# Three small TensorE operations cut from full 128-wide shapes to the rows and columns that they use

## The chip, the cores and the metric

The kernel runs on one core of a Trainium2 chip. The metric is the device time of one execution in microseconds (us); lower is better. Engines are named PE (TensorE, with PEld for its weight loads), DVE (VectorE), ACT (ScalarE), POOL (GpSimd) and SP (the queue that issues DMAs).

## The reference

Three parts follow one another. Only the first is touched by the change; here it is, cut to what matters:

```python
# q, k, v: (2, 8, 768, 64) fp32, proj: (64, 6)
q_bucket = bits of (q @ proj > 0);  k_bucket = bits of (k @ proj > 0)
mask = q_bucket[..., :, None] == k_bucket[..., None, :]
scores = where(mask, q @ k.T / 8, -1e9)
scores = scores - max(scores, axis=-1)
attn = exp(scores) / (sum(exp(scores)) + 1e-9)
out = attn @ v                      # 16 heads of 768 x 64
```

Then come `h = max(x@w1, x@w2, x@w3) @ w_out` on 1536 tokens of 512, and an ELU feed-forward network of width 2048.

## The kernel before

All matmuls keep fp32 accuracy by splitting a value into a high part (`fp32r`) and the low remainder, and running three products. In the program this gives triples such as L623, L624, L625.

The attention part handles 16 heads, one per "slot". A slot has 12 steps (6 tiles of 128 keys times 2 halves of 384 queries), and work on several heads is interleaved: in slot s the scores of head s are made (`scores`, L608 and L609, two matmuls a step), the row maxima of head s+1 (`maxima`, L596, 12 a slot), and the weighted values of half 1 of head s-1 and half 0 of head s (`weigh`, L623 to L625, one triple a step). PE executes its queue in the order in which `emit` (L635) writes it; every cross-engine dependence is a semaphore. Slots 4 to 11 are a hardware loop of two passes over four slots, the others are written out.

Three small operations are in question:

- **The turn of the maxima** (L654, once a slot, after step 8). DVE's L485 leaves the maximum of each query row in 12 columns of `row_max`, a tile of 128 columns; the other 116 are zeros from a memset at the start. PE transposes the whole 128x128 tile; DVE's L499 then reads the 12 rows that matter.
- **The sum of the values** (L659, once a slot, right behind it). A matrix of ones, 128x128, times `val_sum` (128x64) puts the sum of all values on 128 partitions; DVE's `value_total` (L541, L543) reads 12 of them.
- **The correction of an empty row** (L632, twice a slot, the last matmul of each half of `weigh`). It adds `total` times `empty` to the accumulated output. Both operands have 128 partitions, of which 14 hold values (12 rows of `ROWS`, one for each of two parts of epsilon); `total` is zero on the others, and these add nothing. Its end (`pv_ready`) lets ACT copy the half out (L357, L358), and PE may begin the next half's accumulation (L623) when that is done.

In the program each matmul also carries the tile of the PE array that it is issued for. It is 128 rows by 64 columns for L625, whose stationary operand has 64 columns, and the full 128 by 128 for every other matmul of the kernel before, L596 with its 96 rows included.

`set_totals` (L425) is DVE's one-time fill of `total`, `empty`, `minus` and `row_max`, in the slot of offset -1; POOL fills `ones` at L323.

Of the kernel before, what the change touches and what calls it, by code (L numbers as in the profile page):

```python
# [28 lines left out]
FP32 = mybir.dt.float32  # L29
FP32R = mybir.dt.float32r  # L30
# [4 lines left out]
B, H, S, D = 2, 8, 768, 64  # L35
# [4 lines left out]
P = 128  # L40
T = S // P
# [81 lines left out]
def attention(nc, q, k, v, proj, w1, w2, w3, xh, xl, raw, wh, wl, banks, w_loaded, w_split, w_ready, f_ready):  # L123
    ctx = ExitStack()
    with ctx:  # L125
# [4 lines left out]
            return ctx.enter_context(nc.semaphore(name))  # L130

        ident = sb("ident", [P, P])
        ones = sb("ones", [P, P])
        neg_block = sb("neg_block", [ROWS, T, P])


# [13 lines left out]

        total = sb("total", [P, 2, 2 * D], FP32R)
        empty = sb("empty", [P, 2, S], FP32R)
        rounded = sb("rounded", [ROWS, D], FP32R)
        minus = sb("minus", [ROWS, 1])

# [14 lines left out]
        p_hi = sb("p_hi", [P, KEPT, HALF], FP32R)  # L172
        p_lo = sb("p_lo", [P, KEPT, HALF], FP32R)
        half_max = sb("half_max", [P, 2, T, 2])
        row_max = sb("row_max", [P, 2, P])
        x = sb("x", [P, 4, HALF])
        inv = sb("inv", [P, 4, HALF])

# [3 lines left out]
        misc = banks[:, RING + 3:, :]  # L182

        turned = {("q", True): misc, ("k", True): banks[:, 0:2, :], ("q", False): misc, ("k", False): misc}
        mt_all = mx_ps[0][:, HALF:HALF + P]
        mt_ps = mt_all[0:ROWS, :]
        sum_all = mx_ps[1][:, HALF:HALF + D]
        sum_ps = sum_all[0:ROWS, :]

        consts = sem("consts")  # L190
        rows_set = sem("rows_set")
# [222 lines left out]
        def _(dve):  # L414
# [10 lines left out]
            def set_totals():  # L425
                dve.memset(empty[:].bitcast(FP32), 1.0).then_inc(rows_set, 1)
                dve.memset(minus[:], -1.0).then_inc(rows_set, 1)
                dve.memset(row_max[:], 0.0).then_inc(rows_set, 1)
                dve.memset(total[:].bitcast(FP32), 0.0).then_inc(rows_set, 1)
                dve.wait_ge(rows_set, 19)  # L430
                dve.memset(minus[0:T, :], 0.0).then_inc(rows_set, 1)
                dve.memset(total[0:ROWS + 2, :, D:2 * D].bitcast(FP32), EPS_LO).then_inc(rows_set, 1)
                dve.wait_ge(rows_set, 21)
                dve.memset(total[0:ROWS + 1, :, D:2 * D].bitcast(FP32), EPS_HI).then_inc(rows_set, 1)
                dve.wait_ge(rows_set, 22)
                dve.memset(total[0:ROWS, :, D:2 * D].bitcast(FP32), 0.0).then_inc(rows_set, 1)
                dve.wait_ge(rows_set, 23)
                dve.memset(total[0:T, :, D:2 * D].bitcast(FP32), float(S)).then_inc(rows_set, 1)

            def low(s, x, n):  # L440
# [19 lines left out]
            def emit(s):  # L460
                m = s.off + 1
                if s.off == FIRST_SLOT + 2:
                    set_totals()
                for n in range(STEPS):
                    if n == MAX_BEFORE[V_AT + 2] and s.has_st:
                        par = s.off % 2
                        dve.wait_ge(vh_done, s.count(1, 1))
                        dve.tensor_tensor(v_lo[:, par, :, :], v_raw[:, par, :, :],
                                          v_hi[:, par, :, 0:D].bitcast(FP32), ALU.subtract).then_inc(vl_done, 1)
                    if n == INV_AT and s.has_unit:  # L470
                        reciprocals(s, 1)

                    if n == (10 if s.off == FIRST_SLOT + 2 else MAX_BEFORE[TP_AT[0] + 3]) and s.has_tp:
                        low(s, "q", 1)
                    if n == MAX_BEFORE[HASH_AT[0] + 1] and s.has_hash:
                        take_bits(s, "q", 1)
                    if n == MAX_BEFORE[HASH_AT[1] + 1] and s.has_hash:
                        take_bits(s, "k", 2)
                    if s.has_max:
                        dve.wait_ge(mx_ready, s.count(STEPS, STEPS + n + 1))  # L480
                        dve.tensor_reduce(half_max[:, m % 2, n // 2, n % 2:n % 2 + 1], mx_ps[n % 2][:, 0:HALF],  # L481
                                          AX.X, ALU.max).then_inc(mx_read, 1)
                if s.has_max:
                    dve.wait_ge(mx_read, s.count(STEPS, 2 * STEPS))
                    dve.tensor_reduce(row_max[:, m % 2, 0:ROWS].rearrange("p (a t) -> p a t", a=2),  # L485
                                      half_max[:, m % 2, :, :].unsqueeze(1).to_broadcast([P, 2, T, 2]), AX.X, ALU.max
                                      ).then_inc(max_done, 1)
                if s.has_unit:
                    reciprocals(s, 0)
                if s.has_st:  # L490
                    value_total(s)
                if s.has_max:

                    dve.wait_ge(mt_ready, s.count(1, 2))
                    if s.off == FIRST_SLOT + 2:
                        dve.wait_ge(consts, 14)
                        dve.wait_ge(rows_set, 24)
                    rows = operands[m % GROUP][96:96 + ROWS, Q1, :]
                    dve.scalar_tensor_tensor(  # L499
                        out=rows.rearrange("p (t n) -> p t n", t=T), in0=mt_ps.unsqueeze(1).to_broadcast([ROWS, T, P]),  # L500
                        scalar=NONE_BELOW, in1=neg_block[:], op0=ALU.max, op1=ALU.mult).then_inc(mrow_done, 1)
                if s.off == FIRST_SLOT:
                    dve.wait_ge(proj_split, 1)
                    dve.tensor_tensor(proj_lo[:], proj_raw[:], proj_hi[:].bitcast(FP32), ALU.subtract
                                      ).then_inc(proj_split, 1)
                if s.has_tp:
                    low(s, "k", 2)
                if s.has_max:
                    value_sum(s)

                    dve.wait_ge(mrow_done, s.count(1, 2))
                    wait(dve, pv_ready, s.count(2))
                    dve.tensor_scalar(empty[0:ROWS, m % 2, :], rows.bitcast(FP32), -0.5 * NONE_BELOW, None, ALU.is_ge
                                      ).then_inc(empty_done, 1)
                if s.off in (HEADS - 1, HEADS + 1):


                    j = max(s.off - HEADS, 0)
                    dve.wait_ge(w_split, j + 1)
                    dve.wait_ge(st_ready, (HEADS - GROUP + 1) * STEPS)  # L520
                    dve.tensor_tensor(wl[:, j, :], raw[:, j, :], wh[:, j, :].bitcast(FP32), ALU.subtract
                                      ).then_inc(w_ready, 1)
# [27 lines left out]
        def _(pe):  # L550
# [84 lines left out]
            def emit(s):  # L635
                for step in range(STEPS):
                    if s.has_st and step % LAG != 1:
                        scores(s, step)
                    if s.has_max:
                        for n in range(MAX_BEFORE[step], MAX_BEFORE[step + 1]):  # L640
                            maxima(s, n)
                    for i, x in enumerate("qk"):
                        if s.has_tp and step == TP_AT[i]:
                            transposes(s, x, i + 1)
                        if s.has_hash and step == HASH_AT[i]:
                            project(s, x, i + 1)
                    if s.has_st and step % LAG == 0:

                        scores(s, step + 1)
                    if s.has_half1 if step < LAG else s.has_half0:  # L650
                        weigh(s, step)
                    if step == TURN_AT and s.has_max:
                        pe.wait_ge(max_done, s.count(1, 2))
                        pe.transpose(mt_all, row_max[:, (s.off + 1) % 2, :], ident[:]).then_inc(mt_ready, 1)  # L654
                    if step == TURN_AT and s.has_st:
                        pe.wait_ge(vsum_done, s.count(1, 1))
                        if s.off == 0:
                            pe.wait_ge(consts, 15)
                        pe.matmul(sum_all, ones[:], val_sum[:], start=True, stop=True).then_inc(sum_ready, 1)  # L659
                if s.off == HEADS:  # L660


                    pe.wait_ge(w_ready, 1)
                    pe.wait_ge(xl_done, HEADS // B)
                    pe.wait_ge(exp_done, HEADS * STEPS)
                    for u, x in EARLY:
                        if (u, x) == (1, 0):
                            pe.wait_ge(w_ready, 2)
                            pe.wait_ge(mrow_done, HEADS)
                            pe.wait_ge(total_done, 2 * HEADS)  # L670
                        expert(pe, banks, wh, wl, xh, xl, u, x, f_ready)
# [424 lines left out]
```

## Time and profile before

| | |
|---|---|
| median of 3 executions | 757.33 us |
| lowest, highest | 757.12, 758.61 us |
| the profiled execution | 758.61 us |
| its span, first to last instruction | 756.8 us |
| mean granted clock of TensorE, share of full speed | 0.98 |

The profile is one execution, the slowest of the three. Its time is 1.8 us more than its span; this lies around the first and last instruction. Attention runs up to about 294 us of the span, the two feed-forward parts behind it. A MATMUL's end in the trace is modelled, so two matmuls in a row overlap in the listing: what a matmul takes of PE is read from the distance of the starts.

### The profile page before, as it was taken

The numbers are of one execution on the slowest core, as the hardware profiler recorded it, in microseconds if no ns is written. First come the engines' busy times: TensorE is split into PE (matmuls) and PEld (weight loads), VectorE is DVE, ScalarE is ACT, GpSimd is POOL, SyncE is SP. The second block draws the span as 40 slices with busy tenths as digits, with TensorE's granted clock in tenths as the row PEclk, the third lists the DMA queues.
The fourth block names the chain that finished last, engine by engine and source line by source line (L and its number), as shares of the span: only waits on it lengthen the run. The fifth ranks groups of instructions, "written<-read, shape, count | busy, mean of one in ns | idle before, by whom it ended". The sixth has DMA issues, their size and how long they took to land.

```text
span 756.8 us, 10421 instructions
## 1 busy us (share of the span) xinstructions
PE 723.3 (96%) x3440; PEld 617.5 (82%) x3440; DVE 386.3 (51%) x611; ACT 406.7 (54%) x802; POOL 387.0 (51%) x348
## 2 busy tenths in 40 slices
PE   4699999989999988999999999999999999999998
PEld 3499988979998877788888888878888888888886
DVE  3677999879898865322222221143434333343433
ACT  1178889868898894122221112165555555565553
POOL 5078889878898997011101001054444444444452
PEclk9599999999999999999999999999999999999999
DMA  6756364563616300211000001032334333343331
GB/s 133 167 136 151 86 134 99 119 152 77 134 29 144 94 1 0 84 42 42 22 0 22 22 21 42 29 108 86 105 92 145 107 100 95 98 153 97 99 98 55
DMA packets 79634, 64.74 MB, mean 86 GB/s; under 512 B 29152, under 2 KB 68832, under 8 KB 79584
## 3 DMA queue, kind: packets, MB, share of 16 engines
q1 hardware_dynamic: 79584, 64.12, 33.1%
q8 instruction: 25, 0.41, 0.2%
q14 instruction: 25, 0.20, 0.1%
HBM read 40.91 MB, written 3.15 MB: 58 GB/s over the span
## 4 chain that ended last, share of the span: by engine, by line
PE 58%; DVE 0%; ACT 0%; issue 0%
PE banks L694 14%; PE banks L696 14%; PE banks L695 14%; PE banks L1037 6%; PE banks L1041 6%; PE banks L1038 6%; DVE g_sb L980 0%; DVE g_sb L976 0%; DVE out_sb L950 0%; ACT gh L935 0%; ACT neg L930 0%
## 5 line engine op out<-in xcount | busy, mean ns | idle before, releaser
L847 POOL TENSOR_TENSOR wl<-raw,wh 128x512 fp32r<-128x512 f32 (+2 forms) x104 | 143.5, 1400 | 300.5 <-ACT wh L863 300.5
L332 POOL TENSOR_TENSOR p_lo<-probs,p_hi 128x384 fp32r<-128x384 f32 x192 | 199.7, 1061 | 52.9 <-ACT p_hi L380 51.6
L694 PE MATMUL banks<-xh,wh 128*128 128x512 f32 x408 | 158.9, 390 | 0.5 <-PEq L125 0.5
L695 PE MATMUL banks<-xl,wh 128*128 128x512 f32 x408 | 158.7, 389 | 0.0
L696 PE MATMUL banks<-xh,wl 128*128 128x512 f32 x408 | 158.7, 389 | 0.0
L379 ACT ACTIVATE probs<-banks 128x384 f32<-128x384 f32 x192 | 95.0, 495 | 39.3 <-PE banks L609 34.1
L481 DVE TENSOR_REDUCE half_max<-banks 128x1 f32<-128x384 f32 x192 | 99.1, 545 | 23.7 <-PE banks L596 22.1
L380 ACT ACTIVATE p_hi<-banks 128x384 fp32r<-128x384 f32 x192 | 94.4, 492 | 0.0
L976 DVE TENSOR_SCALAR g_sb<-banks 128x512 f32<-128x512 f32 x48 | 33.2, 692 | 119.8 <-ACT neg L930 119.8
L694 PEld LDWEIGHTS banks<-xh,wh 128*128 128x128 f32 x408 | 76.6, 188 | 17.0 <-issue 0.9
L695 PEld LDWEIGHTS banks<-xl,wh 128*128 128x128 f32 x408 | 76.6, 188 | 15.9
L696 PEld LDWEIGHTS banks<-xh,wl 128*128 128x128 f32 x408 | 76.5, 188 | 15.8
L1037 PE MATMUL banks<-wh,gh 128*128 128x512 f32 x192 | 74.9, 390 | 0.2 <-ACT gh L935 0.2
L1041 PE MATMUL banks<-wh,gl 128*128 128x512 f32 x192 | 74.9, 390 | 0.0
L1038 PE MATMUL banks<-wl,gh 128*128 128x512 f32 x192 | 74.7, 389 | 0.0
L623 PE MATMUL banks<-p_hi,v_hi 128*128 128x384 f32 x192 | 67.1, 350 | 7.9 <-ACT inv L358 7.9
L863 ACT ACTIVATE wh<-raw 128x512 fp32r<-128x512 f32 (+2 forms) x104 | 64.6, 665 | 2.6 <-PE banks L1041 0.3
L625 PE MATMUL banks<-p_hi,v_lo 128*64 128x384 f32 x192 | 65.8, 343 | 0.0
L624 PE MATMUL banks<-p_lo,v_hi 128*128 128x384 f32 x192 | 65.5, 341 | 0.0
L930 ACT ACTIVATE neg<-banks 128x512 f32<-128x512 f32 x48 | 28.7, 598 | 68.2 <-PE banks L696 68.2
L909 ACT ACTIVATE hh<-e 128x512 fp32r<-128x512 f32 x18 | 11.4, 632 | 92.4 <-DVE e L960 92.4
L935 ACT ACTIVATE gh<-g_sb 128x512 fp32r<-128x512 f32 x48 | 30.3, 632 | 40.8 <-DVE g_sb L980 40.8
(107 smaller groups left out, 1188.3 us busy)
## 6 DMA issues: line engine op xcount, KB each, us to landing
operands<-wh SPq DMA_DIRECT2D x36, 384.0 KB, 6.9
raw<-in_moe_w_in SPq DMA_DIRECT2D x48, 256.0 KB, 2.6
raw<-in_moe_w_out SPq DMA_DIRECT2D x48, 256.0 KB, 2.7
wl<-wh SPq DMA_DIRECT2D x12, 384.0 KB, 6.4
raw<-in_moe_w SPq DMA_DIRECT2D x18, 256.0 KB, 3.9
q_raw<-in_q SPq DMA_DIRECT2D x16, 192.0 KB, 3.6
k_raw<-in_k SPq DMA_DIRECT2D x16, 192.0 KB, 4.0
v_raw<-in_v SPq DMA_DIRECT2D x16, 192.0 KB, 2.4
```

The costliest lines, as they stand in the source:

```text
L332: pool.tensor_tensor(p_lo[:, at, :], probs[:, step % RING, :], p_hi[:, at, :].bitcast(FP32), ALU.subtract).then_inc(pl_done, 1)
L379: act.activation(probs[:, step % RING, :], scores, ACT.Exp, scale=SCALE)
L380: act.activation(p_hi[:, (STEPS * s.off + step) % KEPT, :], scores, ACT.Exp, scale=SCALE).then_inc(exp_done, 1)
L481: dve.tensor_reduce(half_max[:, m % 2, n // 2, n % 2:n % 2 + 1], mx_ps[n % 2][:, 0:HALF], AX.X, ALU.max).then_inc(mx_read, 1)
L623: pe.matmul(out, v_hi[:, h % 2, kt, :], p_hi[:, kept, :], start=(kt == 0), stop=False)
L694: pe.matmul(out, sh, mh, start=first, stop=False)
L695: pe.matmul(out, sh, ml, start=False, stop=False)
L696: last = pe.matmul(out, sl, mh, start=False, stop=final)
L847: pool.tensor_tensor(wl[:, j, at:at + cols], raw[:, j, at:at + cols], wh[:, j, at:at + cols].bitcast(FP32), ALU.subtract).then_inc(w_ready, 1)
L1037: pe.matmul(acc[t], gh[:, n % 2, cols], w2h, start=(k == 0), stop=False)
L1038: pe.matmul(acc[t], gh[:, n % 2, cols], w2l, start=False, stop=False)
L1041: last = pe.matmul(acc[t], gl[:, n % 2, cols], w2h, start=False, stop=(k == M2 - 1))
```

## The change

`ones` becomes 128x12 and L659 writes 12 partitions. `row_max` becomes 2 buffers of 2x6 columns, and the transpose L654 has a stationary operand of 12 columns and writes 12 partitions. `total` and `empty` get 14 partitions, so that L632 has 14 rows in both operands and still 128 columns. `set_totals` loses the memset of `row_max`, and fills `total` in one memset less; the numbers of the semaphore `rows_set` follow. The count and the order of PE's instructions as written are the same.

```diff
-        ones = sb("ones", [P, P])
+        ones = sb("ones", [P, ROWS])
-        total = sb("total", [P, 2, 2 * D], FP32R)
-        empty = sb("empty", [P, 2, S], FP32R)
+        total = sb("total", [ROWS + 2, 2, 2 * D], FP32R)
+        empty = sb("empty", [ROWS + 2, 2, S], FP32R)
-        row_max = sb("row_max", [P, 2, P])
+        row_max = sb("row_max", [P, 2, 2, T])
-        mt_all = mx_ps[0][:, HALF:HALF + P]
-        mt_ps = mt_all[0:ROWS, :]
-        sum_all = mx_ps[1][:, HALF:HALF + D]
-        sum_ps = sum_all[0:ROWS, :]
+        mt_ps = mx_ps[0][0:ROWS, HALF:HALF + P]
+        sum_ps = mx_ps[1][0:ROWS, HALF:HALF + D]
...
             def set_totals():
                 dve.memset(empty[:].bitcast(FP32), 1.0).then_inc(rows_set, 1)
                 dve.memset(minus[:], -1.0).then_inc(rows_set, 1)
-                dve.memset(row_max[:], 0.0).then_inc(rows_set, 1)
-                dve.memset(total[:].bitcast(FP32), 0.0).then_inc(rows_set, 1)
+                dve.memset(total[:, :, 0:D].bitcast(FP32), 0.0).then_inc(rows_set, 1)
+                dve.memset(total[:, :, D:2 * D].bitcast(FP32), EPS_LO).then_inc(rows_set, 1)
                 dve.wait_ge(rows_set, 19)
                 dve.memset(minus[0:T, :], 0.0).then_inc(rows_set, 1)
-                dve.memset(total[0:ROWS + 2, :, D:2 * D].bitcast(FP32), EPS_LO).then_inc(rows_set, 1)
+                dve.memset(total[0:ROWS + 1, :, D:2 * D].bitcast(FP32), EPS_HI).then_inc(rows_set, 1)
                 dve.wait_ge(rows_set, 21)
-                dve.memset(total[0:ROWS + 1, :, D:2 * D].bitcast(FP32), EPS_HI).then_inc(rows_set, 1)
+                dve.memset(total[0:ROWS, :, D:2 * D].bitcast(FP32), 0.0).then_inc(rows_set, 1)
                 dve.wait_ge(rows_set, 22)
-                dve.memset(total[0:ROWS, :, D:2 * D].bitcast(FP32), 0.0).then_inc(rows_set, 1)
-                dve.wait_ge(rows_set, 23)
                 dve.memset(total[0:T, :, D:2 * D].bitcast(FP32), float(S)).then_inc(rows_set, 1)
...
-                        pe.transpose(mt_all, row_max[:, (s.off + 1) % 2, :], ident[:]).then_inc(mt_ready, 1)
+                        pe.transpose(mt_ps, row_max[:, (s.off + 1) % 2, :, :].rearrange("p a t -> p (a t)"),
+                                     ident[:]).then_inc(mt_ready, 1)
...
-                        pe.matmul(sum_all, ones[:], val_sum[:], start=True, stop=True).then_inc(sum_ready, 1)
+                        pe.matmul(sum_ps, ones[:], val_sum[:], start=True, stop=True).then_inc(sum_ready, 1)
```

## Rows read from the trace of the kernel before

**Rows 1.** Page, part 1: busy time of each engine, share of the span, instructions.
```profile
PE 723.3 (96%) x3440; PEld 617.5 (82%) x3440; DVE 386.3 (51%) x611; ACT 406.7 (54%) x802; POOL 387.0 (51%) x348
```

**Rows 2.** Busy time by stretch: start-up, attention, tail of attention, feed-forward; then clock, DMA.
```profile
18.00:32.00 14.00, 8.82 (x24) 5.72 (x24) 7.10 (x13) 1.62 (x2) 0.00 (x0) 0.50 0.88 201
47.00:300.00 253.00, 241.32 (x1354) 221.77 (x1353) 210.96 (x333) 209.35 (x476) 223.71 (x216) 0.99 0.41 94
157.00:177.00 20.00, 17.39 (x90) 16.03 (x90) 15.04 (x25) 12.80 (x31) 14.41 (x15) 0.91 0.54 120
270.00:294.00 24.00, 19.54 (x98) 17.00 (x98) 11.79 (x14) 17.86 (x41) 22.66 (x21) 0.93 0.00 1
310.00:757.00 447.00, 443.40 (x1952) 365.46 (x1950) 148.96 (x215) 184.00 (x301) 143.54 (x104) 1.00 0.26 74
```

**Rows 3.** Waits from 47 to 300 us: who for whom, total us, times, longest.
```profile
PE banks L623 <- ACT inv L358: 7.9, 11, 2.4
PE banks L596 <- DVE half_max L481: 3.1, 11, 0.5
```

**Rows 4.** PE in order of time, around one L654 and L659: start us, us, instruction.
```profile
109.70 0.33 PE L624 MATMUL banks<-p_lo,v_hi 128*128 128x384 f32 x1
109.88 0.33 PE L625 MATMUL banks<-p_hi,v_lo 128*64 128x384 f32 x1
110.05 0.27 PE L654 MATMUL banks<-ident,row_max 128*128 128x128 f32 x1
110.16 0.33 PE L659 MATMUL banks<-val_sum,ones 128*128 128x64 f32 x2
110.30 0.42 PE L608 MATMUL banks<-wl 128*128 128x384 f32 x1
110.56 0.34 PE L609 MATMUL banks<-wl 128*128 128x384 f32 x1
```

**Rows 5.** Weight loads of the same stretch.
```profile
110.05 0.30 PEld L659 LDWEIGHTS banks<-val_sum,ones 128*128 128x128 f32 x2
110.27 0.19 PEld L608 LDWEIGHTS banks<-wl 128*128 128x128 f32 x1
110.38 0.19 PEld L609 LDWEIGHTS banks<-wl 128*128 128x128 f32 x1
```

**Rows 6.** Lines L625 and L632 over the span: ns min/median/max, starts, shapes.
```profile
L625 PEld LDWEIGHTS banks<-p_hi,v_lo x192: 133/134/223, 45.7 to 293.7; 128*64 128x64 f32 x192
L625 PE MATMUL banks<-p_hi,v_lo x192: 331/337/522, 45.8 to 294.0; 128*64 128x384 f32 x192
L632 PEld LDWEIGHTS banks<-empty,total x32: 187/188/189, 50.4 to 294.0; 128*128 128x128 f32 x32
```

**Rows 7.** PE in order of time, around one L632.
```profile
112.65 0.33 PE L624 MATMUL banks<-p_lo,v_hi 128*128 128x384 f32 x1
112.82 0.33 PE L625 MATMUL banks<-p_hi,v_lo 128*64 128x384 f32 x1
112.99 0.34 PE L632 MATMUL banks<-empty,total 128*128 128x384 f32 x1
113.17 0.34 PE L608 MATMUL banks<-operands 128*128 128x384 f32 x1
```

**Rows 8.** PE and its loads where a matmul begins after a wait.
```profile
289.35 0.44 PE L623 MATMUL banks<-p_hi,v_hi 128*128 128x384 f32 x1 [2.42 <-ACT inv L358]
289.63 0.34 PE L624 MATMUL banks<-p_lo,v_hi 128*128 128x384 f32 x1
...
289.35 0.19 PEld L623 LDWEIGHTS banks<-p_hi,v_hi 128*128 128x128 f32 x1 [2.74 <-ACT inv L358]
289.46 0.19 PEld L624 LDWEIGHTS banks<-p_lo,v_hi 128*128 128x128 f32 x1
```

**Rows 9.** DVE in order of time at the start-up fill, and PE's next matmul.
```profile
16.06 0.27 DVE L428 MEMSET row_max<- 128x256 f32 x1
16.33 0.27 DVE L429 MEMSET total<- 128x256 f32 x1
16.69 0.17 DVE L432 MEMSET total<- 14x128 f32 x1
17.43 0.17 DVE L438 MEMSET total<- 6x128 f32 x1
18.64 1.02 DVE L481 TENSOR_REDUCE half_max<-banks 128x1 f32<-128x384 f32 x2 [1.05 <-PE banks L596]
...
17.92 1.01 PE L596 MATMUL banks<-wl 96*128 96x384 f32 x2 [4.23 <-DMA wl<-bits]
```

**Rows 10.** Lines L654 and L659 over the span; POOL's fill of `ones`.
```profile
L654 PE MATMUL banks<-ident,row_max x16: 270/270/476, 32.3 to 269.5; 128*128 128x128 f32 x16
L659 PE MATMUL banks<-val_sum,ones x32: 218/248/275, 47.7 to 283.8; 128*128 128x64 f32 x32
10.14 0.21 POOL L323 MEMSET ones<- 128x128 f32 x1
```

More of the change, by code:

```diff
@@ L484, in emit @@
                     dve.wait_ge(mx_read, s.count(STEPS, 2 * STEPS))
-                    dve.tensor_reduce(row_max[:, m % 2, 0:ROWS].rearrange("p (a t) -> p a t", a=2),
+                    dve.tensor_reduce(row_max[:, m % 2, :, :],
                                       half_max[:, m % 2, :, :].unsqueeze(1).to_broadcast([P, 2, T, 2]), AX.X, ALU.max
@@ L496, in emit @@
                         dve.wait_ge(consts, 14)
-                        dve.wait_ge(rows_set, 24)
+                        dve.wait_ge(rows_set, 23)
                     rows = operands[m % GROUP][96:96 + ROWS, Q1, :]
```

## Prediction

> **What bounds the kernel now.** I read the totals first: PE is busy for 723.3 of 756.8 us, no other engine for more than 54% [rows 1]. Then the same by stretch, because the change touches attention alone: from 47 to 300 us PE is busy 241.3 of 253 us, from 310 us on 443.4 of 447 [rows 2]. Both stages are bound by PE's queue. In attention PE's idle time has two causes that the list of waits names: 7.9 us at the first matmul of a half, which waits for ACT to have copied the last half out, and 3.1 us at the maxima [rows 3]. So a nanosecond added to or taken from PE in attention passes almost fully into the time, and the question is what PE pays for the three small operations, in distances between starts.
>
> In the steady stream one matmul of 384 columns follows another after 0.17 to 0.18 us, with its load hidden under its predecessor [rows 4, 7]; I use 0.175.
>
> **Part 1: the turn of the maxima and the sum (L654, L659).** From the start of L654 (110.05) to the start of L609 (110.56) PE takes 0.51 us [rows 4]. What sets the pace is the loads: the first of L659 begins at 110.05, that of L608 at 110.27, that of L609 at 110.38 [rows 5], so four loads of 128 columns begin at a distance of 0.11 us each, and then L608 streams its 0.175. The two records of L659 move 64 columns each, which at the rate of the long ones (0.175 us for 384) is 0.03 us; L654 moves 128, 0.06 us. With 12 columns the two loads of L659 shrink: a load of 128 columns is recorded as 0.188 us and one of 64 as 0.134 [rows 6], 0.84 ns a column, so 116 columns less are 0.10 us each. Not both are won, since L608's load still has 128 columns and can start only when the last L659 has begun: 0.06 + 0.03 + 0.11 + 0.175 = 0.37 us to L609's start, 0.14 less than now. The other end is no gain at all, if a short matmul needs as much room as a load. I take 0.11, one load, as the value nearest to a row. L654 and L659 each come 16 times (L659 in two records) [rows 10], side by side but for the first L654 and the last L659; that last L659 lies in the tail of attention, where PE waits for others (19.5 busy of 24 us [rows 2]), so 15 pairs count: 15 x 0.11 = 1.65 us, bounds 0 and 15 x 0.14 = 2.1.
>
> These two are now issued for a part of the array's columns. The trace shows what such a switch costs, 192 times: L625 has 64 columns between matmuls of 128, and starts 0.18 us after L624 and 0.17 us ahead of the next [rows 4, 7]. A switch of columns costs nothing that can be seen, so I add nothing for it. The Trainium skill says otherwise (TensorEngine Tiling (Array Packing), Key Properties): changing the tiling mode, not just the tile, drains TensorE. For columns this case's trace disagrees, with these same distances.
>
> **Part 2: the correction matmul (L632).** It streams 384 columns before and after, and its load keeps 128 columns, so its own length stays at 0.175 us. On the load, the Trainium skill (TensorE: Matmul & The Clock Gate, LDWEIGHTS) says that the columns count and not the rows; no run shows a load of 14 rows, and by the page the load would be neither shorter nor longer. What is new is that the operation needs 14 rows and so can be issued for a group of the array's rows, between matmuls that use all of them. The kernel before has no such operation: 96 rows go to the full array. Its cost is bounded from rows. Below: nothing, as for L625 [rows 7]; there is no gain, since the stream is already continuous. Above: PE finishes the matmul in flight and then loads: a matmul is recorded as 0.34 us where its stream takes 0.175, which leaves 0.165 of pipeline, and a load that isn't hidden adds 0.105 (L623 at 289.35 to L624 at 289.63 is 0.28 us against 0.175 [rows 8]); 0.27 us in all. Between them lies the case where only the load is not drawn ahead over the switch: 0.105 us. That has a row of its own and I take it. Each L632 has a switch in front and one behind, 32 x 2 = 64 of them: 64 x 0.105 = 6.7 us; bounds 0 and 64 x 0.27 = 17.3. The price in front also delays `pv_ready`, so ACT's copy and the next half's first matmul; that wait keeps its length and all moves together, so nothing hides it. In the tail, where POOL is busy for 22.7 of 24 us [rows 2], four L632 may be covered (0.8 us), which I leave inside the range.
>
> **Part 3: the fill at the start.** DVE loses the memset of `row_max` (0.27 us) and has two of 128 columns (0.17 each) for one of 256 and one of 128 (0.27 and 0.17) [rows 9]: 0.37 us less. It then idles for 1.05 us until PE's L596, which is held to 17.92 by the DMA of the hash bits [rows 9]. The fill ends at 17.6 at the latest, so the gain is covered: 0, and -0.37 at most if it were not. POOL's fill of `ones`, at 10.1 us, has its first reader at 47.7 [rows 10]. DVE's readers (L499, L541, L543) touch 12 partitions as before. The smaller tiles move the addresses of those behind them; no row prices this, and I take 0.
>
> **The sum.** -1.65 + 6.7 + 0 = +5.1 us. On the profiled execution that is 758.61 + 5.1 = 763.7; this one is the slowest of three, 1.28 above the median, so against the median I forecast 757.33 + 5.1 = 762.4 us. Its own range, with 0.05 to 0.17 us a switch, is +1.5 to +9.2: 758.9 to 766.6.
>
> **The rivals.**
>
> A. *No price for a group of rows.* L632 behaves as L625 does and the narrower loads of L659 remain: -1.65 (0 to -2.1), 755.7 us. For it: 192 switches of columns cost nothing [rows 6, 7]. [...] This is the case on the other side; it decides as soon as a switch of rows costs under 1.65 / 64 = 0.026 us.
>
> B. *A full drain at each switch of rows.* 17.3 - 1.65 = +15.7, 773.0 us. For it: L632 adds into the same bank as the L625 in front of it, so its sum must not overtake. Against it: the free switches of L625, which adds into that bank too. The rule on the tiling mode quoted above would give this case.
>
> C. *The narrow transpose loses its single pass.* L654 is one record of fp32, L659 two [rows 4]. If the transpose with 12 columns ran as an ordinary fp32 matmul it would have two records as well, the second at the distance of a load, 0.11 us: 16 x 0.11 = 1.8 us, which eats the gain of part 1. Without a price for rows the time is then 757.5, no change. The Trainium skill has this as a rule (TensorEngine Tiling (Array Packing), Feature Incompatibilities): column tiling excludes the transpose mode for fp32. Nothing in the trace before bears on it, as all its transposes are 128 wide.
>
> D. *The clock.* In the two stretches where PE waited for 2 us and more at once, the mean granted clock was 0.91 and 0.93 [rows 2]. Stalls of 0.1 to 0.3 us make no such wait, and over the whole of 47 to 300 us, with 11 waits of up to 2.4 us at L623, the mean was 0.99 [rows 2, 3]: one more such dip, 0.1 off the clock for 20 us, is worth 2 us at most. I put it at nothing and inside the range.
>
> **How the numbers follow.** The forecast (some price at each switch of rows, less than a drain) 0.52; A 0.24; C without a price for rows 0.12; B 0.12. What a measurement of this kernel can tell from no change is 0.2%, 1.5 us. The forecast is slower but for its lowest edge (0.49 of 0.52) and so is B: together 0.61. A lies around the bound, so it splits: 0.17 faster by more, and the rest, 0.07, with C and the edge makes 0.22 for no change. The range runs from A, with its 2.1 us all but taken, to above the forecast's own range, and leaves out B: 755.4 to 769.
>
> **What would show it.** L609 starting 0.37 to 0.40 us after L654, with L659's loads recorded at some 0.09 us: part 1 right. One L654 record a slot: C wrong; two: C right. The start of L632 after L625, and of L608 after L632: 0.175 both, A; near 0.28, the forecast, with the load of L632 or of its successor beginning after the predecessor's stream; 0.44, B. PE's busy count from 310 us on must stay as it is. The forecast is wrong if both distances at L632 stay at 0.175, or if a stall appears at L654 or L659, where L625's rows say that there is none.

## The result: 768.97 us against 757.23, and the profile after

The changed kernel takes 768.97 us (median of 4, 768.22 to 770.23), the kernel before 757.23 (median of 4): ratio 1.0154, 95% interval 1.0134 to 1.0174, so +11.7 us (+10.1 to +13.2). The direction was forecast, the size was not: +5.1 us was predicted, and +11.7 lies above the forecast's own range (up to 766.6); 768.97 is at the upper edge of the whole range of 755.4 to 769.

The profiled execution of the changed kernel took 768.09 us, with a span of 766.3; that is 9.5 us more than the profiled execution of the kernel before (758.61), because the one is the fastest execution of its kernel and the other the slowest. In its code the lines of attention have moved up: L619 to L621 are the old L623 to L625, L628 is L632, L604 and L605 are L608 and L609, L650 and L656 are L654 and L659. First the two stages, cut where the first expert matmul starts (294.33 us before, 303.73 after): span, busy PE, PEld, DVE, ACT, POOL, then clock, DMA share and GB/s. The kernel before:

```profile
47.00:294.30 247.30, 235.62 (x1329) 217.05 (x1328) 206.51 (x330) 206.47 (x472) 221.24 (x214) 0.99 0.42 96
294.30:756.80 462.50, 458.59 (x2018) 377.76 (x2016) 154.33 (x219) 188.00 (x307) 148.05 (x107) 1.00 0.25 72
```

The changed kernel:

```profile
47.00:303.70 256.70, 247.76 (x1322) 211.96 (x1321) 206.71 (x329) 207.40 (x471) 218.73 (x213) 0.99 0.41 92
303.70:766.30 462.60, 458.68 (x2017) 377.96 (x2016) 154.25 (x219) 188.10 (x307) 148.70 (x108) 1.00 0.25 72
```

The feed-forward parts are as long as before, to 0.1 us; attention is 9.4 us longer. PE is counted busy 12 us longer in it, DVE and ACT as long as before to 1 us and POOL 2.5 us less, at the same clock. Weight loads are busy 5 us less. So the time went to PE's matmuls, and not to the length of its loads.

Around a correction matmul (to be read against [rows 7]; PE, then its loads):

```profile
98.15 0.34 PE L621 MATMUL banks<-p_hi,v_lo 128*64 128x384 f32 x1
98.42 0.44 PE L628 MATMUL banks<-empty,total 14*128 14x384 f32 x1
98.78 0.44 PE L604 MATMUL banks<-wl 128*128 128x384 f32 x1
99.06 0.34 PE L605 MATMUL banks<-wl 128*128 128x384 f32 x1
...
98.41 0.18 PEld L628 LDWEIGHTS banks<-empty,total 14*128 14x128 f32 x1 [0.30 <-issue]
98.78 0.19 PEld L604 LDWEIGHTS banks<-wl 128*128 128x128 f32 x1 [0.19 <-issue]
98.89 0.19 PEld L605 LDWEIGHTS banks<-wl 128*128 128x128 f32 x1
```

From L621 to L605 it is 0.91 us, against 0.53 from L625 to L609, the same four matmuls, in the kernel before ([rows 7] has the first three). Look at the loads: that of L628 begins at 98.41 together with its matmul; in the kernel before the stream runs on at 0.175 us, with the load hidden under L625. It is 0.26 us behind L621's start, 0.085 after the end of L621's stream (0.175). The load of L604 is again 0.085 after L628's stream (98.42 + 0.105 of load + 0.175 = 98.70). Each switch thus costs 0.085 us of waiting and 0.105 of a load that no stream hides, 0.19 us. 30 of the 32 have this distance to 0.01 us; one is 0.05 longer, and the last also runs into the wait at the end of attention. The median is 0.385 above that of the kernel before: 32 x 0.385 = 12.3 us.

Around the transpose and the sum (to be read against [rows 4, 5]):

```profile
95.00 0.34 PE L621 MATMUL banks<-p_hi,v_lo 128*64 128x384 f32 x1
95.17 0.27 PE L650 MATMUL banks<-ident,row_max 128*12 128x128 f32 x1
95.38 0.28 PE L656 MATMUL banks<-val_sum,ones 128*12 128x64 f32 x2
95.59 0.44 PE L604 MATMUL banks<-operands 128*128 128x384 f32 x1
95.87 0.33 PE L605 MATMUL banks<-operands 128*128 128x384 f32 x1
...
95.00 0.09 PEld L650 LDWEIGHTS banks<-ident,row_max 128*12 128x12 f32 x1
95.38 0.10 PEld L656 LDWEIGHTS banks<-val_sum,ones 128*12 128x12 f32 x2 [0.29 <-issue]
95.59 0.19 PEld L604 LDWEIGHTS banks<-operands 128*128 128x128 f32 x1
```

The loads did shrink as worked out (0.09 us for 12 columns), but from L650 to L605 it is 0.70 us, not 0.51: +0.19 a slot, 15 x 0.19 = 2.9 us lost where 1.65 were to be won. L650 itself starts 0.17 us after L621 with its load ahead; the stall stands in front of L656 and behind it. The lines over the whole span (ns min/median/max; the list of waits from 47 to 300 us below it):

```profile
L628 PEld LDWEIGHTS banks<-empty,total x32: 181/181/182, 49.8 to 303.4; 14*128 14x128 f32 x32
L628 PE MATMUL banks<-empty,total x32: 433/436/438, 49.8 to 303.4; 14*128 14x384 f32 x32
L650 PE MATMUL banks<-ident,row_max x16: 270/273/381, 31.7 to 279.2; 128*12 128x128 f32 x16
```

```profile
PEld banks L628 <- issue: 9.4, 31, 0.3
PEld banks L656 <- issue: 4.5, 15, 0.5
PE banks L619 <- ACT inv L356: 3.1, 3, 1.9
```

The two "issue" rows are the stalls: the profile shows no semaphore that holds these loads. And PE's waits for ACT at the first matmul of a half fell from 7.9 us in 11 waits [rows 3] to 3.1 in 3, or 4.2 in 4 if the list is taken up to 304 us, the end of attention here: a part of what PE lost in stalls it no longer waits.

### The profile page after: what moved, and what is told of

It reads as the page before. It is cut to its first block, busy times and chain, and to the rows that moved or that the text cites. A ratio compares the mean times of both kernels' runs of the same rounds, so it can differ in the third digit from the quotient of the medians.

```text
span 766.3 us, 10420 instructions
## 1 busy us (share of the span) xinstructions
PE 735.5 (96%) x3440; PEld 612.4 (80%) x3440; DVE 386.2 (50%) x610; ACT 408.4 (53%) x802; POOL 385.8 (50%) x348
## 4 chain that ended last, share of the span: by engine, by line
PE 58%; DVE 0%; ACT 0%; issue 0%
PE banks L691 14%; PE banks L693 14%; PE banks L692 14%; PE banks L1034 6%; PE banks L1038 6%; PE banks L1035 6%; DVE g_sb L977 0%; DVE g_sb L973 0%; DVE out_sb L947 0%; ACT gh L932 0%; ACT neg L927 0%
## 5 line engine op out<-in xcount | busy, mean ns | idle before, releaser
L619 PE MATMUL banks<-p_hi,v_hi 128*128 128x384 f32 x192 | 66.7, 347 | 4.2 <-ACT inv L356 4.2
L621 PE MATMUL banks<-p_hi,v_lo 128*64 128x384 f32 x192 | 65.4, 341 | 0.0
L604 PE MATMUL banks<-operands 128*128 128x384 f32 x144 | 53.8, 374 | 0.4 <-ACT p_hi L378 0.4
```

The source lines that it names most:

```text
L619: pe.matmul(out, v_hi[:, h % 2, kt, :], p_hi[:, kept, :], start=(kt == 0), stop=False)
```

## The experiments

Each is the kernel before with the one edit shown. Distances are medians over the heads, and an interval of a ratio is one of 95%; the triple distance runs from the 128x64 matmul in front of the correction to the second full matmul behind it (0.53 us before), the pair distance from the transpose to the second full matmul behind the sum (0.51 us before).

**rows14** (only the correction):

```diff
-        total = sb("total", [P, 2, 2 * D], FP32R)
-        empty = sb("empty", [P, 2, S], FP32R)
+        total = sb("total", [14, 2, 2 * D], FP32R)
+        empty = sb("empty", [14, 2, S], FP32R)
```

> Only total and empty have 14 partitions; ones and row_max stay 128 wide. Theory S (each switch between a group of rows and the full array costs PE 0.085 us of waiting and a weight load of 0.105 us that is no longer hidden): from the start of the 128x64 matmul before it to the start of the second full matmul behind it 0.91 us against 0.525, so +0.385 for each of 32, up to +12.3 us, of which the waits for ACT absorb a part: +8 to +12 us. Theory C (the narrow columns of the transpose and of the ones matmul are the dear part): +0 to +2 us.

Ratio 1.0087 (1.0065 to 1.0110), +6.6 us; the triple distance is 0.91 us to 0.01 in 30 of the 32 (one is 0.10 longer, the last runs into the wait at the end of attention), the pair distance 0.51. The stall is the rows' own, but the time is below what was expected of it: 12.3 us are lost at these places and 6.6 arrive. The wait for ACT from 47 to 300 us shows where a part of the rest is:

```profile
PE banks L623 <- ACT inv L358: 5.2, 4, 2.2
```

It was 7.9 in 11 waits [rows 3]. Adding up over attention all distances between starts of PE's matmuls that exceed the stream by over 0.12 us, the places of the correction, the transpose and the sum left out, gives 16.4 us before and 11.6 here: 4.8 us of waits are gone. By the same count the four kernels with 14 or 64 rows (the changed kernel, rows14, rows64, halves14) have 9.9 to 12.8 us, and the ten without 16.4 to 21.7. So the stalls of the rows do shorten PE's other waits.

**rows96** (the same with 96 partitions, which the program issues for the full array):

```diff
-        total = sb("total", [P, 2, 2 * D], FP32R)
-        empty = sb("empty", [P, 2, S], FP32R)
+        total = sb("total", [96, 2, 2 * D], FP32R)
+        empty = sb("empty", [96, 2, S], FP32R)
```

> total and empty have 96 partitions, of which 82 add zeros; the program issues the matmul for the full array. Theory S (the array tile counts): the distances stay at 0.175 us and the time at that of the kernel before, within 0.2%. Theory R (any matmul with fewer rows than its neighbours pays): +8 to +12 us as with 14 rows, or in proportion to the rows left out, +3 us.

Ratio 1.0006 (0.9990 to 1.0022), triple distance 0.53 us. With 96 rows in the operand nothing is lost as long as the tile is the full array; theory R falls.

**rows64** (64 partitions, a tile of 64 by 128):

```diff
-        total = sb("total", [P, 2, 2 * D], FP32R)
-        empty = sb("empty", [P, 2, S], FP32R)
+        total = sb("total", [64, 2, 2 * D], FP32R)
+        empty = sb("empty", [64, 2, S], FP32R)
```

> total and empty have 64 partitions; the matmul is issued for an array tile of 64 rows by 128 columns. Theory S for every partial group of rows: the same 0.19 us a switch as with 14 rows, +8 to +12 us. Rival F (only a group of 32 rows costs, as a tile of 64 columns is free while the neighbours are full): no change within 0.2%.

Ratio 1.0100 (1.0078 to 1.0123), +7.6 us, triple distance 0.92:

```profile
91.43 0.33 PE L625 MATMUL banks<-p_hi,v_lo 128*64 128x384 f32 x1
91.69 0.44 PE L632 MATMUL banks<-empty,total 64*128 64x384 f32 x1
92.06 0.45 PE L608 MATMUL banks<-operands 128*128 128x384 f32 x1
92.35 0.34 PE L609 MATMUL banks<-operands 128*128 128x384 f32 x1
```

The medians of the three steps are 0.27, 0.37 and 0.28, those of 14 rows to 0.01. So a group of 64 rows costs what one of 32 costs; rival F falls. A fourth execution took 1845 us and is not in the ratio; nothing on record says why.

**halves14** (rows14 with the correction cut in two):

```diff
-                    pe.matmul(out, total[:, h % 2, :], empty[:, h % 2, half:half + HALF], start=False, stop=True
-                              ).then_inc(pv_ready, 1)
+                    mid = HALF // 2
+                    pe.matmul(pv_ps[:, 0:mid], total[:, h % 2, :], empty[:, h % 2, half:half + mid],
+                              start=False, stop=False)
+                    pe.matmul(pv_ps[:, mid:HALF], total[:, h % 2, :], empty[:, h % 2, half + mid:half + HALF],
+                              start=False, stop=True).then_inc(pv_ready, 1)
```

> As rows14, with the matmul of 14 rows cut in two of 192 columns each that follow one another. Theory S (a price per switch of the array tile, not per matmul of few rows): 0.27 us from the 128x64 matmul to the first half, then 0.11 us (the load of the second half sets the pace), 0.28 from the second half, 0.28 behind: 0.93 to 0.95 us in all against 0.91, and the time of rows14 within 0.2%. Rival M (each matmul of a group of rows pays, and can't be drawn ahead of the one in flight): 0.19 us more for each of 32, +2 to +6 us over rows14.

Ratio 1.0088 (1.0070 to 1.0107), that of rows14.

```profile
91.32 0.33 PE L625 MATMUL banks<-p_hi,v_lo 128*64 128x384 f32 x1
91.58 0.35 PE L633 MATMUL banks<-empty,total 14*128 14x192 f32 x1
91.77 0.27 PE L635 MATMUL banks<-empty,total 14*128 14x192 f32 x1
91.97 0.44 PE L608 MATMUL banks<-operands 128*128 128x384 f32 x1
92.25 0.34 PE L609 MATMUL banks<-operands 128*128 128x384 f32 x1
...
91.58 0.18 PEld L633 LDWEIGHTS banks<-empty,total 14*128 14x128 f32 x1 [0.29 <-issue]
91.69 0.19 PEld L635 LDWEIGHTS banks<-empty,total 14*128 14x128 f32 x1
```

Twice as many matmuls of 14 rows take 0.93 us here (median 0.94), not 1.1: the load of the second half begins 0.11 us after that of the first, ahead of its own matmul as in the full stream. The price is one per switch, not per matmul; rival M falls.

**cols12** (only the transpose and the sum):

```diff
-        row_max = sb("row_max", [P, 2, P])
+        row_max = sb("row_max", [P, 2, 12])
-        ones = sb("ones", [P, P])
+        ones = sb("ones", [P, 12])
-        mt_all = mx_ps[0][:, HALF:HALF + P]
+        mt_all = mx_ps[0][0:12, HALF:HALF + P]
-        sum_all = mx_ps[1][:, HALF:HALF + D]
+        sum_all = mx_ps[1][0:12, HALF:HALF + D]
```

> Only ones and row_max have 12 columns; total and empty stay at 128 partitions. From the start of the transpose to the start of the second full matmul behind the pair 0.70 us against 0.51, so +0.19 a slot for 15 slots: +2.9 us at most, +2 to +3 if nothing absorbs it. Theory N (narrow loads alone, with the stall of the changed kernel coming from the rows): -1.6 us.

Ratio 1.0048 (1.0032 to 1.0063), +3.6 us, pair distance 0.69, triple distance 0.53. This part is a loss by itself, and the loss is near the 2.9 us of 15 x 0.19. The two parts alone make +10.2 us, the change +11.7, alike within their intervals.

**turn12 and ones12** (one of the two each; the diffs are the halves of cols12):

> Only the transpose has 12 columns. In the changed kernel it starts 0.175 us after the 128x64 matmul, and what follows it comes 0.20 us later instead of 0.11, with its load not ahead. Theory L (the price is paid on leaving a 32-column tile): 0.20 us from the transpose to the ones matmul or a little more, then the old pattern, +0.1 to +0.2 us a slot, +1.5 to +3 us. Theory G (the price is that of the ones matmul): 0.11 and 0.14 and 0.26 as before, no change.

> Only the ones matmul has 12 columns, behind a full transpose. Theory L: its load is drawn ahead of its start, and the full matmul behind it pays 0.085 us and an open load of 0.105 us: 0.50 to 0.60 us from the transpose to the second full matmul against 0.51, 0 to +1.4 us. Theory G: most of the +0.19 us a slot, +2.9 us.

turn12: ratio 1.0006 (0.9995 to 1.0018), pair distance 0.51. ones12: ratio 1.0047 (1.0029 to 1.0064), pair distance 0.69. PE and its loads, first turn12, then ones12:

```profile
92.76 0.34 PE L625 MATMUL banks<-p_hi,v_lo 128*64 128x384 f32 x1
92.93 0.27 PE L654 MATMUL banks<-ident,row_max 128*12 128x128 f32 x1
93.04 0.33 PE L659 MATMUL banks<-val_sum,ones 128*128 128x64 f32 x2
...
92.94 0.30 PEld L659 LDWEIGHTS banks<-val_sum,ones 128*128 128x128 f32 x2
```

```profile
93.46 0.27 PE L654 MATMUL banks<-ident,row_max 128*128 128x128 f32 x1
93.66 0.28 PE L659 MATMUL banks<-val_sum,ones 128*12 128x64 f32 x2
93.87 0.44 PE L608 MATMUL banks<-operands 128*128 128x384 f32 x1
94.15 0.34 PE L609 MATMUL banks<-operands 128*128 128x384 f32 x1
...
93.66 0.10 PEld L659 LDWEIGHTS banks<-val_sum,ones 128*12 128x12 f32 x2 [0.23 <-issue]
```

The transpose of 12 columns changes no distance, neither in front of it nor behind it. The whole stall belongs to the sum. Theory L, which laid it on leaving a tile of 32 columns and so on the transpose as well, falls; G holds.

**ones64** (the sum with 64 columns):

```diff
-        ones = sb("ones", [P, P])
+        ones = sb("ones", [P, 64])
...
-        sum_all = mx_ps[1][:, HALF:HALF + D]
+        sum_all = mx_ps[1][0:64, HALF:HALF + D]
```

> Only the ones matmul is narrow, with 64 columns, a tile of 128 by 64 like that of the value matmul whose switches are free. If tiles of 64 columns are free for plain fp32 too, its two loads are shorter by 0.05 us each and the transpose-to-second-full distance falls from 0.51 to 0.41 to 0.46 us; if leaving any tile of part of the columns costs in fp32, it rises to 0.55 us or more.

Pair distance 0.74 us; one execution, 761.34 us. 64 columns stall as 12 do, and the two loads are longer by 0.04 us each. So it isn't the width alone: L625 has 64 columns, too, and pays nothing.

**vlo32** (192 switches to a tile of 32 columns, in fp32r; half of the low product is left out):

```diff
-                pe.matmul(pv_ps[0:D, 0:HALF], v_lo[:, h % 2, kt, :], p_hi[:, kept, :], start=False, stop=False
+                pe.matmul(pv_ps[0:D // 2, 0:HALF], v_lo[:, h % 2, kt, 0:D // 2], p_hi[:, kept, :], start=False, stop=False
```

> The low product of the values uses 32 of its 64 columns and writes 32 partitions instead of 64 (half of the low product is left out); the program issues it for a tile of 128 by 32, in fp32r, 192 times. Theory T (partial columns are free for fp32r operands and for transposes, dear for plain fp32): 0.175 us before and behind it, the time as before within 0.2%. Rival W (a tile of 32 columns is dear in itself): 0.385 us for each of 192, +30 us and more.

```profile
92.65 0.33 PE L624 MATMUL banks<-p_lo,v_hi 128*128 128x384 f32 x1
92.82 0.34 PE L625 MATMUL banks<-p_hi,v_lo 128*32 128x384 f32 x1
93.00 0.34 PE L608 MATMUL banks<-operands 128*128 128x384 f32 x1
```

The medians of the 192 are 0.176 us in front and 0.175 behind. The one execution took 760.13 us, 0.3% over the median of the kernel before and at the upper end of its range, where rival W asked for 30 us more.

**ones12r** (the sum with 12 columns and both operands in fp32r, the sum of the values rounded by it):

```diff
-        ones = sb("ones", [P, P])
+        ones = sb("ones", [P, 12], FP32R)
...
-        val_sum = sb("val_sum", [P, D])
+        val_sum = sb("val_sum", [P, D], FP32R)
...
-        sum_all = mx_ps[1][:, HALF:HALF + D]
+        sum_all = mx_ps[1][0:12, HALF:HALF + D]
```

> The ones matmul with 12 columns, as in ones12, but both operands in fp32r instead of fp32, so one record instead of two and the sum of the values rounded. Theory T: no stall; its load is ahead of its start, the transpose is followed after 0.11 us or less, and the distance from the transpose to the second full matmul is 0.40 us or less. Rival (narrow and short is dear in every type): the transpose is followed after 0.20 us, the load behind it begins 0.085 us after its stream, 0.60 us or more in all.

```profile
93.59 0.27 PE L655 MATMUL banks<-ident,row_max 128*128 128x128 f32 x1
93.62 0.27 PE L660 MATMUL banks<-val_sum,ones 128*12 128x64 f32 x1
93.73 0.42 PE L609 MATMUL banks<-operands 128*128 128x384 f32 x1
93.99 0.33 PE L610 MATMUL banks<-operands 128*128 128x384 f32 x1
...
93.59 0.09 PEld L660 LDWEIGHTS banks<-val_sum,ones 128*12 128x12 f32 x1
93.70 0.19 PEld L609 LDWEIGHTS banks<-operands 128*128 128x128 f32 x1
```

0.40 us in all, no stall. With 12 columns in both, plain fp32 pays and fp32r doesn't. The one execution took 762.93 us in spite of it; a single time is worth little here (the kernel before ran from 756.12 to 760.02 in all). In its trace attention ends 4.3 us later than in that of the kernel before, and by the count of rows14 PE's other long distances sum to 21.7 us instead of 16.4. So it waited more at other places; the runs don't show why.

**cols72 and small** (no switch that had a price). cols72 gives `ones` and `row_max` 72 columns, which the program issues for the full array; small takes 12 columns for the transpose, 72 for the sum and 96 rows for the correction.

> Transpose and ones matmul have 72 columns, which the program issues for the full array, so that the loads are shorter without a switch. Theory S: no stall; the loads of the ones matmul take 0.06 us each instead of 0.107, the distance from the transpose to the second full matmul falls from 0.51 to about 0.42 us, and the time by 15 x 0.09 = 1.3 us, about the resolution of 0.2%. If the narrow load itself were the cause of the stall, the distance rises.

> The best of the parts: 12 columns for the transpose (free in turn12), 72 columns for the ones matmul and 96 rows for the correction, all of them without a priced switch. The pair takes 0.46 us as in cols72 against 0.51, the correction 0.53; the time is 0.7 us below the kernel before, ratio 0.998 to 1.000.

The pair in cols72:

```profile
91.31 0.27 PE L654 MATMUL banks<-ident,row_max 128*72 128x128 f32 x1
91.42 0.28 PE L659 MATMUL banks<-val_sum,ones 128*72 128x64 f32 x2
91.52 0.42 PE L608 MATMUL banks<-operands 128*128 128x384 f32 x1
91.78 0.33 PE L609 MATMUL banks<-operands 128*128 128x384 f32 x1
```

Pair distance 0.46 us in both, less than before but not the 0.42 expected of cols72. Against this pair without a stall, those of ones12 and ones64 take 0.23 and 0.28 us more, way in and way out together. Ratios 0.9990 (0.9978 to 1.0001) and 0.9987 (0.9971 to 1.0003): a gain of 0.8 to 1.0 us that the runs can't tell from none. So nothing that can be told from noise came out of the change's idea.

## Why the prediction was wrong in size

- **What bounds the kernel: right, with one step too far.** In the profiled executions the difference is in attention and at PE, and the stage behind is equal to 0.1 us. But time added to PE did not pass "almost fully" into the total: of 12.3 us only 6.6 did (rows14).
- **Part 1 failed, at "a switch of columns costs nothing that can be seen, so I add nothing for it".** -1.65 us was taken, between 0 and -2.1; alone this part measured +3.6 (+2.4 to +4.8), and 2.9 by the distances. It was read from 192 switches of L625, and for L625, which is fp32r, it holds down to 32 columns (vlo32). L659 is plain fp32, and there the pair takes 0.19 us more with 12 columns (0.18 in ones12). The Trainium skill (TensorEngine Tiling (Array Packing), Key Properties) says that a change of the tiling mode drains TensorE; the trace of L659 agrees as far as a stall goes, that of L625 and vlo32 shows none. Rows of one operand type were carried over to another. This step is 5.3 of the 6.6 us that the sum missed.
- **The gain inside part 1 was also too large.** It took L654 as 0.06 us of stream. In ones12r the load of L609 begins 0.11 us after the transpose starts though only a load of 12 columns lies between; in cols72, with loads of 72 columns, the sum still follows the transpose after 0.11. I infer that the transpose holds PE for 0.11 itself. Without a switch the gain is 0.05 us a slot (cols72), 0.7 us, not 1.65.
- **Part 2: half of the mechanism was right, two steps were wrong, and they cancel.** The load that is no longer drawn ahead over the switch is there, with its 0.105 us. What the chosen case left out is the wait of 0.085 us in front of that load: the term "64 x 0.105 = 6.7" measured 32 x 0.385 = 12.3 at the matmuls. "So nothing hides it" was wrong as well: about half of this (5.7 us) did not arrive, and 4.8 us of shorter waits at other places account for most of that. What is left is 6.6 us (rows14), beside the 6.7 of the forecast. That agreement is luck: the three steps from L625 to L609 take 0.27, 0.37 and 0.28 us, where 0.28, 0.28 and 0.175 were forecast.
- **Rival B, the full drain, fits the lines best, priced too high.** A load of 128 columns is recorded for 0.19 us while such loads follow one another after 0.11; I take the first 0.08 of the record as time in which the array isn't yet touched. The load of L628 is issued at 98.41, and 98.41 + 0.08 is 98.49, which is where L621 is recorded to end (98.15 + 0.34). The same holds behind: 98.78 + 0.08 = 98.86 = 98.42 + 0.44. And it holds at the sum: L650 is recorded to end at 95.17 + 0.27 = 95.44, and the load of L656 gives 95.38 + 0.08 = 95.46. So at the correction 0.165 of pipeline + 0.105 of load - 0.08 that overlap = 0.19. The upper bound of 0.27 left out this overlap. That the array empties is inferred from these coincidences, and the recorded ends are modelled; the runs show the price of a group of rows and that it falls once per switch.
- **Rival C fell:** L650 is one record of 0.27 us with 12 columns, and turn12 costs nothing. The rule of the Trainium skill that column tiling excludes the fp32 transpose (TensorEngine Tiling (Array Packing), Feature Incompatibilities) shows no price here. One reading is that the partial tile isn't put into effect for transposes and fp32r, which would also make L625 and vlo32 free. For the transpose cols12 speaks for it: there the transpose and the sum are both issued for a tile of 128 by 32, so no switch would stand between them, and yet the sum follows after 0.20 us, as behind the full transpose of ones12, while its own two records follow one another after 0.06. For fp32r no run tells this reading apart from a switch that costs nothing.
- **A fell** with the first distance. **Part 3 and D held:** the clock is 0.99 in attention in both, and after its shorter fill DVE only waits longer for PE, 1.63 us instead of 1.05.

## What to carry to other kernels

Don't trim a small matmul to its used rows between full ones: with 14 and with 64 rows it was issued for a group of rows and cost 0.19 us on the way in and again on the way out, while zeros up to 96 or 128 rows were free. In plain fp32 few columns cost, too: the pair with the sum took 0.18 us more with 12 columns and 0.23 with 64, way in and way out together. Fp32r matmuls of 12, 32 and 64 columns and a transpose of 12 columns had no such price. Stalls of this kind show as weight loads that begin with their matmul after "issue", and what they cost in time is their sum less the waits that they swallow, so price both from rows of the same operand type.

## What was not expected of the hardware

One and the same shape, 128 by 12 or by 64, costs no stall in fp32r, and 0.18 to 0.23 us in all in plain fp32. And about half of 12.3 us of stalls on an engine that is busy for 95% of the stage came back as shorter waits of that engine: a busy share near 1 doesn't mean that all that is added arrives.
